# Two steps of an attention pair turned in one visit of TensorE, and five changes of order

## The chip, the cores and the metric

One core of a Trainium2 chip runs the whole program. The time is in microseconds (us) of the device for one execution. Lower is better. The engines are TensorE (PE, with its weight loads PEld), VectorE (DVE), ScalarE (ACT), GpSimd (POOL) and SyncE (SP), which only issues DMAs here.

## What is computed

```python
# attention: q, k, v are (4, 8, 576, 64); each position sees itself and the 63 before it
scores = np.matmul(q, k.transpose(0, 1, 3, 2)) / np.sqrt(D)
attn = softmax(np.where((rel >= 0) & (rel < 64), scores, -1e9))   # sum + 1e-9 below the line
x = np.matmul(attn, v)                                            # as 2304 tokens x 512
# first layer
x = ((x @ w1) * (x @ w2)) @ w3 @ w_out                            # 512 -> 1024 -> 1024 -> 512
# second layer
h = x @ w_in                                                      # 512 -> 2048
out = np.maximum(0.01 * h, h) @ w_out2                            # 2048 -> 512
```

## The kernel before

**Products.** w3 @ w_out is multiplied out first, so the first layer is two products, an elementwise one and a third. Every large product is cut into halves of both sides and done as seven block products P1 to P7 in place of eight, with sums of blocks before and behind. Each operand is split into a rounded part (hi, copied by ACT) and the rest (lo, subtracted by DVE), and a block product is three passes hi*hi, hi*lo, lo*hi (`three_passes`, lines 403 to 407). Tokens go in three chunks of 768.

**Stages.** The first stage makes w3 @ w_out in 16 slots (`wprod_slot`), each of 12 matmuls of 512 columns; its inputs come in pieces (`PIECES`), which ACT copies (`split_piece`, L818) and DVE subtracts (L1181). Then come 168 slots of the list `AB_SEQ`, twelve rounds r of 14 block products: slot n is one product of six matmuls of 384 columns (`ab_product`). `slot_of(r, m)` is the number of a slot; from round 1 on m runs from -1 to 12. Behind these come the third product of the first layer (`y_product`) and the two of the second layer.

**Attention** is laid between these slots. It has 36 steps g of 64 queries each, twelve per chunk; chunk 0 belongs to the first stage, chunk 1 to slots 5 to 47, chunk 2 to slots 62 to 104. Two steps, g even and g + 1, form a pair. In slots counted from the scores of a step (`SCORES[g]`, three slots between the steps of a pair, six from pair to pair), step g goes:
- scores of both steps of the pair on PE (L1695) at the end of the even one's slot;
- DVE scales and masks (L1225), and takes the row maximum (L1230), one slot later, for each step on its own;
- ACT's exponentials (L840) two and three slots later;
- DVE inverts the sums (`invert_sums`, L1240) four slots later, behind its work on that slot's product, and POOL multiplies the probabilities by them (`normalize`, L770);
- PE turns the probabilities with four transposes (`turn`, L1685) in the middle of the product eight slots later (`TURN`), into the bank `ps_more`; ACT copies them out (`turn_copy`, L834);
- PE multiplies with the values (`values`, L1675) for the pair, at the end of the slot nine behind the odd step's scores (`VALUES`), into the bank `ps_values`; ACT (in the first stage DVE) copies that out one slot later (`values_copy`).
In the first stage the numbers are 2 for the turn and 3 for the values.

**Order.** Each engine runs its instructions in the order in which the loops write them, and a wait on a semaphore holds everything behind it on that engine. There is no planner: the places of side work in slots are tables by hand (`AB_SUMS`, POOL's sums for weight unit f; `AB_HI` and `AB_LO`, ACT's and DVE's halves of the split of a unit; `XS_HI_NEXT` and `XS_LO_NEXT`, the same for blocks of x in rounds 4 and 8, where "t3" is a sum of x-parts on DVE). The banks of products are handed on by `bank_waits`: P6 waits for c11 (DVE, L1328), P2 for c21 of the round before (DVE, L1390). SP issues loads and stores in one queue; `store_p` and `store_p_late` write a round's three results.

Of the kernel before, what the change touches and what calls it, by code (L numbers as in the profile page):

```python
# [78 lines left out]
for _c in range(2):  # L79
    for _j in range(CSTEPS):  # L80
        SCORES[(_c + 1) * CSTEPS + _j] = slot_of(4 * _c, 5 + 3 * _j)
EXPS_A, EXPS_B, RECIP, TURN, VALUES = 2, 3, 4, 8, 9


SCORED, VALUED = {}, {}
for _g in range(NSTEP):
    SCORED[_g] = SCORES0[_g - _g % 2] if _g < CSTEPS else SCORES[_g - _g % 2]
    VALUED[_g] = SCORES0[_g | 1] + VALUES0 if _g < CSTEPS else SCORES[_g | 1] + VALUES

PIECES = []  # L90
# [33 lines left out]
def unit_of(f):  # L124
    if f < F_WSUM:
        return f
    if f < F_IN:
# [10 lines left out]
P0_HI = {2: (0, 0), 3: (0, 1), 5: (1, 0), 6: (1, 1), 9: (2, 0), 10: (2, 1), 12: (3, 0), 13: (3, 1)}  # L138
P0_LO = {3: (0, 0), 4: (0, 1), 6: (1, 0), 8: (1, 1), 10: (2, 0), 11: (2, 1), 13: (3, 0), 14: (3, 1)}
AB_LOAD = {(0, 2): (4,), (0, 6): (5,), (0, 10): (6,), (1, 1): (7,), (9, -1): (8, 9), (10, -1): (10, 11), (11, 8): (12, 13)}  # L140
AB_SUMS = {slot_of(0, 7): 4, slot_of(0, 10): 5, slot_of(1, 1): 6, slot_of(1, 4): 7}
AB_HI = {(1, 0): (4, 0), (1, 2): (4, 1), (1, 4): (5, 0), (1, 8): (5, 1),
# [3 lines left out]
AB_LO = {(1, 1): (4, 0), (1, 4): (4, 1), (1, 5): (5, 0), (1, 11): (5, 1),  # L146
# [3 lines left out]

XS_HI_FIRST = {2: P6, 3: P3, 4: P7, 7: P4}
XS_HI_LAST = {3: P2, 5: P1, 8: P5, 12: P6}
XS_HI_NEXT = {1: P3, 2: P7, 7: P4}
XS_LO_FIRST = {0: "t2", 1: "t3", 2: P6, 4: P3, 5: P7, 6: "t4", 8: P4}
XS_LO_LAST = {4: P2, 6: P1, 7: "t1", 9: P5, 11: "t2"}
XS_LO_NEXT = {-1: P6, 0: "t3", 3: P3, 4: P7, 5: "t4", 8: P4}

TYEARLY = 10
TY_LOAD = {(9, 6): (0, 1), (10, 3): (2, 3), (10, 8): (4, 5), (11, 2): (6, 7), (11, 5): (8, 9), (11, 9): (TYEARLY + 2,), (11, 11): (TYEARLY + 3,)}
# [56 lines left out]
def build(nc, qk_steps, v_steps, masks, w3, wo, w12, w_in, w_out, out):  # L216
    with ExitStack() as ctx:
# [75 lines left out]
        ps_scores = [ps_pair[:, :].rearrange("p (h b k) -> p h b k", h=HP, b=2)[:, :, b] for b in range(2)]  # L293
        ps_more = ctx.enter_context(nc.psum_tensor("ps_more", [P, 512], F32))
        ps_v = ctx.enter_context(nc.psum_tensor("ps_values", [P, 512], F32))
        ps_turned = ps_more[:, :].rearrange("p (h k) -> p h k", h=HP)
        ps_heads = ps_v[:, :].rearrange("p (h b q) -> p h b q", h=HP, b=2)

        wsum_dram = nc.dram_tensor("wsum_between", (KF, P, DM), F32, kind="Internal").ap()
# [23 lines left out]

        piece_in = [sem(f"piece_in{i}") for i in range(PRAW)]
        piece_hi = sem("piece_hi")
        piece_lo = sem("piece_lo")
        wprod_used = sem("wprod_used")
        wsum_done = [sem(f"wsum_done{i}") for i in range(4)]
# [80 lines left out]
        def bank(r, i, s):  # L409

            if r < AR:
                return (acc[s], acc[2 + s], acc[s], acc[s], acc[s], acc[2 + s], acc[s])[i]
            alpha = ((ps_s, ps_t), (acc[2], acc[3]))[r % 2][s]
            gamma, beta = (ps_v, ps_more)[s], acc[s]
            return (alpha, gamma, alpha, beta, alpha, gamma, alpha)[i]

        def piece_dest(i, part):

# [80 lines left out]
        def _(sp):  # L499
# [179 lines left out]
            for n in range(NSEQ):  # L679
                r = AB_SEQ[n][0]  # L680
                m = n - slot_of(r, 0)
                for g in range(CSTEPS + 2, NSTEP):
                    if SCORED[g - 2] == n - 1:
                        load_qk(g)
                    if VALUED[g - 2] == n - 1:
                        load_v(g)
                if r > 0 and m == 3:
                    store_p(r - 1)
                    store_p_late(r - 1)
                for f in AB_LOAD.get((r, m), ()):  # L690
                    load_fill(f)
                for u in range(NPRE):
                    if PRE_STORE[u] == n:
                        store_pre(u)
                    if PRE_LOAD[u] == n:
                        load_pre(u)
                for k in TY_LOAD.get((r, m), ()):
                    load_ty(k)
# [113 lines left out]
        def _(act):  # L812
# [18 lines left out]

            def turn_copy(g):
                act.wait_ge(turned, g + 1)
                act.activation(probs[g % 4], ps_turned, ACT.Copy).then_inc(pt_done, 1)  # L834

            def exps(g, pairs):
                r, w = g % 2, width(g)
# [134 lines left out]
            for i in (1, 3):  # L972
                act.dma_start(piece_raw[i], wo[PIECES[i][1]]).then_inc(piece_in[i], 16)
            act.dma_start(mask_s[:, :], masks).then_inc(mask_in, 16)
            for i in pieces_for(0):
                split_piece(i)
            for k in range(WSLOTS):
                for g in range(CSTEPS):
                    if SCORES0[g] + TURN0 == k - 1:
                        turn_copy(g)  # L980
                for i in pieces_for(k + 1):
                    split_piece(i)
                for g in range(CSTEPS):
                    if SCORES0[g] == k - 1:
                        exps(g, range(HP))
                if k in P0_HI:
                    split_fill(*P0_HI[k])
                if k == KF - 1:
                    save_wsum(0, 0)
                    save_wsum(0, 2)  # L990
                if k == WSLOTS - 5:
                    split_x(0, P2)
                if k == WSLOTS - 3:
                    split_x(0, P1)
# [4 lines left out]
            for n, (r, i, s) in enumerate(AB_SEQ):  # L999
                q, m = r // ROUNDS, n - slot_of(r, 0)  # L1000
                for g in range(CSTEPS, NSTEP):
                    if SCORES[g] + TURN == n:
                        turn_copy(g)
                    if g % 2 == 0 and VALUED[g] == n - 1:
                        values_copy(g)
# [170 lines left out]
        def _(dve):  # L1176
            dve.memset(probs[0][:, :, BQ:KW], 0.0).then_inc(probs_zero, 1)

            def split_piece(i):
                dve.wait_ge(piece_hi, i + 1)  # L1180
                dve.tensor_tensor(piece_dest(i, 1), piece_raw[i % PRAW], piece_dest(i, 0).bitcast(F32),  # L1181
                                  ALU.subtract).then_inc(piece_lo, 1)

# [275 lines left out]
                dve.tensor_tensor(lo, t_source(k), hi.bitcast(F32), ALU.subtract).then_inc(t_lo, 1)  # L1459


            for i in pieces_for(0):
                split_piece(i)
            for k in range(WSLOTS - 1):
# [201 lines left out]
        def _(pe):  # L1666
            def values(g):
                pe.wait_ge(v_in[g % 2], 16 * (g // 2 + 1))
                pe.wait_ge(pt_done, g + 1)
                pe.wait_ge(x_done, g - g % 2)  # L1670
                for h in range(H):
                    d = slice(h % 2 * D, (h % 2 + 1) * D)
                    w = slice(h * D, (h + 1) * D)
                    turned_at = (h ^ (h >= H // 2)) * BQ
                    last = pe.matmul(ps_heads[d, h // 2, g % 2], v_raw[:, g % 2, w],  # L1675
                                     pt[g % 4][:, turned_at:turned_at + BQ], start=True, stop=True)
                last.then_inc(values_done, 1)

            def turn(g):
                if g == 0:  # L1680
                    pe.wait_ge(probs_zero, 1)
                pe.wait_ge(probs_done, g + 1)
                pe.wait_ge(pt_done, g)
                for u in range(HP):
                    last = pe.transpose(ps_turned[:, u], probs[g % 4][:, u], ident[:, :])  # L1685
                last.then_inc(turned, 1)

            def scores(g):
# [10 lines left out]
            def attention_first(k):  # L1699
# [4 lines left out]
                    if SCORED[g] == k:  # L1704
                        scores(g)
                for g in range(CSTEPS):
                    if SCORES0[g] + TURN0 == k:
                        turn(g)

            def attention(n):  # L1710
# [6 lines left out]

            def first_slot():
                w, m_hi, m_lo = w3_ring[0], wo_s[:, 0, 0], wo_s[:, 0, 1]
                pe.wait_ge(piece_hi, 2)  # L1720
                for m in range(4):
                    pe.matmul(acc[m][:, :], w[:, 0, m * P:(m + 1) * P], m_hi, start=True, stop=False)
                    if m == 0:
# [58 lines left out]

            def turns(k):
                for g in range(CSTEPS, NSTEP):
                    if SCORES[g] + TURN == k:
                        turn(g)

            def ab_product(k, r, i, s):
# [161 lines left out]
```

## Time and profile before

| | us |
|---|---|
| median of 3 runs | 733.97 |
| lowest, highest | 733.32, 737.0 |
| the profiled execution, in all | 732.78 |
| its span in the trace | 730.9 |
| PE busy (share of the span) | 721.8 (99%) |
| PE's weight loads | 697.3 (95%) |
| DVE busy | 530.2 (73%) |
| ACT busy | 417.5 (57%) |
| POOL busy | 101.2 (14%) |
| granted clock of TensorE | 1.000 of full speed |

The span reaches from the first to the last instruction of the trace; the rest of the execution's time lies around it. PE's matmuls are shown with a modelled end, and one is shown as running when the next has begun: a row of 0.33 us is followed by the next start 0.17 us later. The starts, not the busy shares, tell whether PE lost time. Where a row ends with a bracket, the engine was idle for that long before it, and the name behind the arrow is what it waited for.

### The profile page before, as it was taken

To read this page: it belongs to the slowest core of one execution; us is meant where nothing else is said; L and a number is where in the kernel's file an instruction comes from. 1 tells how busy PE (TensorE), PEld (TensorE's weight loads), DVE (VectorE), ACT (ScalarE), POOL (GpSimd) and SP (SyncE) were. 2 spreads that over 40 slices of the span, in tenths; PEclk is the share of its full clock that TensorE was granted. 3 is DMA by queue.
4 is the path that set the end of the run, shared out by engine and by line. 5 is a ranking of instruction groups with operands and counts; after the bars stand their busy time and mean duration, and the time that the engine had idled before them with its cause. 6 is when DMAs were issued, how large, how long until landed. Compare 5 with 4: busy or idle time off the path is not lost.

```text
span 730.9 us, 13803 instructions
## 1 busy us (share of the span) xinstructions
PE 721.8 (99%) x5032; PEld 697.3 (95%) x5032; DVE 530.2 (73%) x833; ACT 417.5 (57%) x889; POOL 101.2 (14%) x122
## 2 busy tenths in 40 slices
PE   8999999999999999999999999999999999999998
PEld 7888899999899999999999999999999999999998
DVE  5988888797767679798778968669789655445452
ACT  5876677646564345656546656456677544544541
POOL 3433564413333110000000000000000000000000
DMA  9884677545654589988857988987996468778773
GB/s 324 296 300 164 208 233 239 190 163 183 197 172 172 184 300 393 313 279 322 296 178 291 323 281 295 359 285 248 377 375 244 130 181 241 206 215 232 207 202 116
DMA packets 96835, 181.13 MB, mean 248 GB/s; under 512 B 7936, under 2 KB 55680, under 8 KB 96768
## 3 DMA queue, kind: packets, MB, share of 16 engines
q1 hardware_dynamic: 90032, 166.62, 68.6%
q10 hardware_dynamic: 6736, 13.63, 5.2%
q8 instruction: 40, 0.66, 0.4%
q14 instruction: 27, 0.22, 0.1%
HBM read 111.80 MB, written 68.42 MB: 247 GB/s over the span
## 4 chain that ended last, share of the span: by engine, by line
PE 62%; ACT 0%; issue 0%; DVE 0%
PE acc L405 10%; PE acc L407 9%; PE acc L406 9%; PE ps_pair L405 5%; PE ps_pair L407 5%; PE ps_pair L406 5%; PE ps_more L407 3%; PE ps_more L405 3%; PE ps_values L405 3%; PE ps_values L407 3%; PE ps_more L406 3%; PE ps_values L406 3%; ACT arena L952 0%; DVE arena L1364 0%
## 5 line engine op out<-in xcount | busy, mean ns | idle before, releaser
L405 PE MATMUL acc<-parts,weights_a 128*128 128x384 f32 (+1 forms) x320 | 112.0, 350 | 0.9 <-DVE arena L1390 0.6
L407 PE MATMUL acc<-parts,weights_a 128*128 128x384 f32 (+1 forms) x320 | 109.5, 342 | 0.0
L405 PE MATMUL acc<-parts,weights_b 128*128 128x384 f32 x320 | 109.1, 341 | 0.3 <-DVE arena L1328 0.3
L406 PE MATMUL acc<-parts,weights_a 128*128 128x384 f32 (+1 forms) x320 | 109.3, 342 | 0.0
L407 PE MATMUL acc<-parts,weights_b 128*128 128x384 f32 x320 | 107.1, 335 | 0.0
L406 PE MATMUL acc<-parts,weights_b 128*128 128x384 f32 x320 | 107.0, 334 | 0.0
L1459 DVE TENSOR_TENSOR parts<-raw_c,parts 128x768 fp32r<-128x768 f32 x64 | 61.2, 958 | 60.2 <-ACT parts L957 60.1
L957 ACT ACTIVATE parts<-raw_c 128x768 fp32r<-128x768 f32 x64 | 54.0, 846 | 67.9 <-DMA raw_c<-g_between 65.5
L405 PEld LDWEIGHTS acc<-parts,weights_a 128*128 128x128 f32 x320 | 60.1, 188 | 5.2 <-issue 2.2
L840 ACT ACTIVATE arena<-arena,negmax 128x128 f32<-128x128 f32 (+1 forms) x144 | 55.2, 386 | 13.3 <-DVE negmax L1230 13.2
L405 PEld LDWEIGHTS acc<-parts,weights_b 128*128 128x128 f32 x320 | 60.1, 188 | 1.8 <-issue 1.2
L407 PEld LDWEIGHTS acc<-parts,weights_a 128*128 128x128 f32 x320 | 60.1, 188 | 1.7
L406 PEld LDWEIGHTS acc<-parts,weights_a 128*128 128x128 f32 x320 | 60.1, 188 | 1.3
L406 PEld LDWEIGHTS acc<-parts,weights_b 128*128 128x128 f32 x320 | 60.1, 188 | 0.0
L407 PEld LDWEIGHTS acc<-parts,weights_b 128*128 128x128 f32 x320 | 60.0, 188 | 0.0
L936 ACT ACTIVATE arena<-arena 128x384 f32<-128x384 f32 x72 | 35.9, 525 | 39.5 <-DVE arena L1328 17.6
L770 POOL TENSOR_TENSOR arena<-arena,rsum 128x512 f32<-128x512 f32 (+1 forms) x36 | 41.1, 1141 | 102.8 <-DVE rsum L1240 102.8
L911 ACT ACTIVATE parts<-arena 128x768 fp32r<-128x768 f32 x42 | 35.3, 848 | 33.9 <-PE ps_pair L407 11.5
L1400 DVE TENSOR_TENSOR parts<-arena,parts 128x768 fp32r<-128x768 f32 x42 | 39.7, 954 | 13.6 <-ACT parts L911 13.5
L1328 DVE TENSOR_TENSOR arena<-acc,arena 128x384 f32<-128x384 f32 x60 | 31.6, 552 | 17.2 <-PE acc L407 13.1
L405 PE MATMUL ps_pair<-parts,weights_b 128*128 128x384 f32 x120 | 40.1, 334 | 0.0
L406 PE MATMUL ps_pair<-parts,weights_b 128*128 128x384 f32 x120 | 40.1, 334 | 0.0
(212 smaller groups left out, 1761.9 us busy)
## 6 DMA issues: line engine op xcount, KB each, us to landing
g_between<-arena SPq DMA_DIRECT2D x75, 384.0 KB, 4.8
raw_c<-g_between SPq DMA_DIRECT2D x64, 384.0 KB, 3.4
arena<-p_between SPq DMA_DIRECT2D x42, 384.0 KB, 5.2
arena<-qk_steps SPq DMA_DIRECT2D x36, 384.0 KB, 5.0
arena<-v_steps SPq DMA_DIRECT2D x36, 256.0 KB, 3.8
p_between<-arena SPq DMA_DIRECT2D x24, 384.0 KB, 4.8
x_between<-arena ACTq DMA_DIRECT2D x21, 384.0 KB, 5.6
arena<-x_between SPq DMA_DIRECT2D x21, 384.0 KB, 5.6
```

Source lines behind the costliest of these rows:

```text
L405: eng.matmul(out_ap, w_hi, m_hi, start=start, stop=False, skip_group_check=resumed)
L406: eng.matmul(out_ap, w_hi, m_lo, start=False, stop=False, skip_group_check=resumed)
L407: return eng.matmul(out_ap, w_lo, m_hi, start=False, stop=stop, skip_group_check=resumed)
L770: pool.tensor_tensor(probs[g % 4][:, :, 0:w], probs[g % 4][:, :, 0:w], rsum[:, r * HP:(r + 1) * HP].unsqueeze(2).to_broadcast([P, HP, w]), ...
L840: act.activation(probs[g % 4][:, u, 0:w], probs[g % 4][:, u, 0:w], ACT.Exp, bias=negmax[:, r * HP + u:r * HP + u + 1], scale=1.0, accum_ou ...
L911: act.activation(block_places[k % NPROD][:, 0:BW], ty_raw[TY_SLOT[k]], ACT.Copy).then_inc(ty_hi, 1)
L936: act.activation(g, g, ACT.Prelu, alpha=SLOPE).then_inc(g_done[q], 1)
L957: act.activation(block_places[k % NPROD][:, 0:BW].rearrange("p (j t) -> p j t", j=2), t_source(k), ACT.Copy).then_inc(t_hi, 1)
L1328: dve.tensor_tensor(dest, bank(r, i, s)[:, 0:CT], p1_sb[:, s], ALU.add).then_inc(c11_done, 1)
L1400: dve.tensor_tensor(b[:, BW:2 * BW], ty_raw[TY_SLOT[k]], b[:, 0:BW].bitcast(F32), ALU.subtract).then_inc(ty_lo, 1)
L1459: dve.tensor_tensor(lo, t_source(k), hi.bitcast(F32), ALU.subtract).then_inc(t_lo, 1)
```

## The change

Both steps of a pair are turned in one visit of PE, in the slot that lies seven behind the odd step's scores (`TURNED`; in the first stage two behind, as before for the odd one). The even step goes to `ps_more` as before, the odd step to `ps_values`, so it waits until the values of the pair before have been copied out of there, and no longer until the even step's copy is done. The values of a pair wait for both copies. ACT copies the two one after the other. The slot of the values is the same.

Besides: POOL's sums for weight unit 5 move three slots back. In rounds 4 and 8 the sum "t3" on DVE moves from m = 0 to 2, and ACT's copy of block P7 from 2 to 3. DVE's parts (10, 1), (11, 0) and (11, 1) of the last weight splits move back. In round 5 SP issues `store_p` and `store_p_late` of the round before one slot later, behind loads. At the start DVE, in place of ACT, makes the hi part of the first piece of w_out.

```diff
-EXPS_A, EXPS_B, RECIP, TURN, VALUES = 2, 3, 4, 8, 9
+EXPS_A, EXPS_B, RECIP, TURN, VALUES = 2, 3, 4, 7, 9
+    TURNED[_g] = SCORES0[_g | 1] + TURN0 if _g < CSTEPS else SCORES[_g | 1] + TURN
@@ tables
-AB_SUMS = {slot_of(0, 7): 4, slot_of(0, 10): 5, slot_of(1, 1): 6, slot_of(1, 4): 7}
+AB_SUMS = {slot_of(0, 7): 4, slot_of(0, 13): 5, slot_of(1, 1): 6, slot_of(1, 4): 7}
-         (10, 6): (10, 0), (10, 11): (10, 1), (11, 1): (11, 0), (11, 4): (11, 1)}
+         (10, 6): (10, 0), (11, 1): (10, 1), (11, 4): (11, 0), (11, 5): (11, 1)}
-XS_HI_NEXT = {1: P3, 2: P7, 7: P4}
+XS_HI_NEXT = {1: P3, 3: P7, 7: P4}
-XS_LO_NEXT = {-1: P6, 0: "t3", 3: P3, 4: P7, 5: "t4", 8: P4}
+XS_LO_NEXT = {-1: P6, 2: "t3", 3: P3, 4: P7, 5: "t4", 8: P4}
@@ build
-        ps_turned = ps_more[:, :].rearrange("p (h k) -> p h k", h=HP)
+        ps_turned = [ps[:, :].rearrange("p (h k) -> p h k", h=HP) for ps in (ps_more, ps_v)]
+        def turned_place(g):
+
+            return ps_turned[g % 2]
@@ SP
-                if r > 0 and m == 3:
+                if r > 0 and m == (4 if slot_of(r, 3) in VALUED.values() else 3):
                     store_p(r - 1)
                     store_p_late(r - 1)
@@ ACT
-                act.activation(probs[g % 4], ps_turned, ACT.Copy).then_inc(pt_done, 1)
+                act.activation(probs[g % 4], turned_place(g), ACT.Copy).then_inc(pt_done, 1)
-            for i in pieces_for(0):
-                split_piece(i)
+            split_piece(0)
-                    if SCORES0[g] + TURN0 == k - 1:
+                    if TURNED[g] == k - 1:
-                    if SCORES[g] + TURN == n:
+                    if TURNED[g] == n:
                         turn_copy(g)
@@ DVE
-                dve.wait_ge(piece_hi, i + 1)
+                if i == 1:
+                    dve.wait_ge(first_hi, 1)
+                else:
+                    dve.wait_ge(piece_hi, max(i, 1))
+            dve.wait_ge(piece_in[1], 16)
+            dve.tensor_copy(piece_dest(1, 0), piece_raw[1]).then_inc(first_hi, 1)
             for i in pieces_for(0):
                 split_piece(i)
@@ PE, values
-                pe.wait_ge(pt_done, g + 1)
+                pe.wait_ge(pt_done, (g | 1) + 1)
@@ PE, turn
-                pe.wait_ge(pt_done, g)
+                if g % 2:
+                    pe.wait_ge(x_done, g - 1)
+                else:
+                    pe.wait_ge(pt_done, g)
@@ PE, first_slot
-                pe.wait_ge(piece_hi, 2)
+                pe.wait_ge(piece_hi, 1)
+                pe.wait_ge(first_hi, 1)
```

## Rows read from the trace of the kernel before

**Rows 1.** Windows: length, busy us of PE, PEld, DVE, ACT, POOL, clock, DMA share, GB/s.

```profile
140.00:190.00 50.00, 48.23 (x461) 45.41 (x460) 37.79 (x70) 26.91 (x81) 11.34 (x14) 1.00 0.58 191
```

**Rows 2.** Waits of PE: engine, tile and line, then releaser, total us, times, longest.

```profile
PE ps_more L1685 <- POOL arena L770: 1.1, 2, 0.9
```

**Rows 3.** Timeline of PE and ACT round one turn: start us, us, engine, line, operation.

```profile
120.18 0.34 PE L407 MATMUL acc<-parts,weights_b 128*128 128x384 f32 x1
120.36 0.60 PE L1685 MATMUL ps_more<-ident,arena 128*128 128x128 f32 x4
120.71 0.42 PE L405 MATMUL acc<-parts,weights_b 128*128 128x384 f32 x1
120.97 0.34 PE L406 MATMUL acc<-parts,weights_b 128*128 128x384 f32 x1
121.67 0.58 ACT L834 ACTIVATE arena<-ps_more 128x512 f32<-128x512 f32 x1
```

**Rows 4.** Timeline of DVE, POOL and PE round the turn of step 13.

```profile
88.18 0.18 DVE L1240 RECIPROCAL rsum<-sums_eps 128x4 f32<-128x4 f32 x1
89.97 1.35 POOL L770 TENSOR_TENSOR arena<-arena,rsum 128x512 f32<-128x512 f32 x1
90.12 0.34 PE L407 MATMUL acc<-parts,weights_a 128*128 128x384 f32 x1
91.37 0.66 PE L1685 MATMUL ps_more<-ident,arena 128*128 128x128 f32 x4 [0.92 <-POOL arena L770]
```

**Rows 5.** Timeline of DVE, POOL and PE round the turn of step 15.

```profile
99.10 1.20 DVE L1193 TENSOR_TENSOR weights_b<-raw_b,weights_b 128x1024 fp32r<-128x1024 f32 x1
99.27 1.93 POOL L770 TENSOR_TENSOR arena<-arena,rsum 128x512 f32<-128x512 f32 x1 [0.34 <-DVE rsum L1240]
99.72 0.33 PE L407 MATMUL acc<-parts,weights_a 128*128 128x384 f32 x1
100.76 0.34 PE L407 MATMUL acc<-parts,weights_a 128*128 128x384 f32 x1
```

**Rows 6.** Timeline of POOL and PE round the turn of step 33.

```profile
209.42 1.04 POOL L770 TENSOR_TENSOR arena<-arena,rsum 128x512 f32<-128x512 f32 x1 [6.27 <-DVE rsum L1240]
211.09 0.60 PE L1685 MATMUL ps_more<-ident,arena 128*128 128x128 f32 x4
```

**Rows 7.** Timeline of PE at two turns of the first stage.

```profile
28.60 0.60 PE L1685 MATMUL ps_more<-ident,arena 128*128 128x128 f32 x4
29.17 0.50 PE L405 MATMUL acc<-parts,weights_a 128*128 128x512 f32 x1
```

**Rows 8.** Timeline of DVE and PE, sixth product of round 4.

```profile
154.99 0.95 DVE L1274 TENSOR_TENSOR arena<-arena 128x768 f32<-128x768 f32 x1
155.96 0.34 PE L407 MATMUL acc<-parts,weights_a 128*128 128x384 f32 x1
156.55 0.41 PE L405 MATMUL acc<-parts,weights_a 128*128 128x384 f32 x1 [0.25 <-DVE arena L1328]
```

**Rows 9.** Timeline of SP's DMA issues and of PE, scores of steps 30 and 31.

```profile
174.68 0.57 SPq L588 DMA_DIRECT2D p_between<-arena  x1
179.40 1.00 SPq L573 DMA_DIRECT2D arena<-qk_steps  x2
186.22 0.67 PE L1695 MATMUL ps_pair<-arena 64*64 64x128 f32 x16 [1.52 <-DMA arena<-qk_steps]
```

**Rows 10.** Timeline of DVE and PE, third product of round 11.

```profile
275.43 1.21 DVE L1193 TENSOR_TENSOR weights_b<-raw_b,weights_b 128x1024 fp32r<-128x1024 f32 x1
276.19 0.34 PE L407 MATMUL acc<-parts,weights_a 128*128 128x384 f32 x1
277.17 0.44 PE L405 MATMUL acc<-parts,weights_a 128*128 128x384 f32 x1 [0.64 <-DVE arena L1390]
```

**Rows 11.** Timeline of DVE and PE at the first products.

```profile
5.48 0.69 DVE L1181 TENSOR_TENSOR weights_a<-arena,weights_a 128x512 fp32r<-128x512 f32 x1 [4.35 <-ACT weights_a L818]
6.36 0.39 PE L1725 MATMUL acc<-parts,weights_a 128*128 128x512 f32 x1
```

More of the change, by code:

```diff
@@ L81 @@
         SCORES[(_c + 1) * CSTEPS + _j] = slot_of(4 * _c, 5 + 3 * _j)
-EXPS_A, EXPS_B, RECIP, TURN, VALUES = 2, 3, 4, 8, 9
-SCORED, VALUED = {}, {}
+EXPS_A, EXPS_B, RECIP, TURN, VALUES = 2, 3, 4, 7, 9
+SCORED, TURNED, VALUED = {}, {}, {}
 for _g in range(NSTEP):
     SCORED[_g] = SCORES0[_g - _g % 2] if _g < CSTEPS else SCORES[_g - _g % 2]
+    TURNED[_g] = SCORES0[_g | 1] + TURN0 if _g < CSTEPS else SCORES[_g | 1] + TURN
     VALUED[_g] = SCORES0[_g | 1] + VALUES0 if _g < CSTEPS else SCORES[_g | 1] + VALUES
@@ L325, in build @@
         piece_hi = sem("piece_hi")
+        first_hi = sem("first_hi")
         piece_lo = sem("piece_lo")
@@ L1682, in turn @@
                 pe.wait_ge(probs_done, g + 1)
-                pe.wait_ge(pt_done, g)
+                if g % 2:
+                    pe.wait_ge(x_done, g - 1)
+                else:
+                    pe.wait_ge(pt_done, g)
                 for u in range(HP):
-                    last = pe.transpose(ps_turned[:, u], probs[g % 4][:, u], ident[:, :])
+                    last = pe.transpose(turned_place(g)[:, u], probs[g % 4][:, u], ident[:, :])
                 last.then_inc(turned, 1)
@@ L1706, in attention_first @@
                 for g in range(CSTEPS):
-                    if SCORES0[g] + TURN0 == k:
+                    if TURNED[g] == k:
                         turn(g)
@@ L1784, in turns @@
                 for g in range(CSTEPS, NSTEP):
-                    if SCORES[g] + TURN == k:
+                    if TURNED[g] == k:
                         turn(g)
```

## The prediction

> **What bounds the kernel now.** I read the stages first, then who made PE wait, then starts on PE's timeline. The windows show PE busy for 48.23 of 50 us in one of the slices with attention work, clock 1.00, nothing else near full [rows 1]: TensorE's own stream is the bound. A matmul's shown length overlaps the next one, so I don't count busy time but starts: two third passes of neighbouring products begin at 99.72 and 100.76, so **a product costs 1.04 us**, 0.173 us a matmul [rows 5]. Every start later than that pace is a stall of the whole kernel. Going through all starts up to 290 us I find eight stalls in the stages that overlap products with attention, 5.1 us together, and some 0.9 us in the first stage; behind 290 us ten short ones sum to 1.0, and the change touches none of them. The wait list names POOL's normalisation twice [rows 2].
>
> **The turn visits.** A visit of four transposes costs: the pass before starts at 120.18, the second after it at 120.97, which is 0.79 us, less two passes (0.35), so 0.44 [rows 3]. Four transposes at 0.11 are that already; entering and leaving cost about 0.02. Twenty-four visits in the product stages become twelve, so joining them gives 12 x 0.02 = **-0.2 us** (between 0 and 18 x 0.1 = 1.8, were the entry as dear as the 0.1 that a visit of values or scores loses on entering; the transposes' own row is the nearer, so 0.2). The same eight transposes are still made.
>
> **The odd step comes one product earlier.** TURN was 8 slots behind each step's own scores; now both go 7 behind the odd one's. The even one gains two slots, the odd one loses one, 1.04 us. The 0.44 of the even transposes was ahead of the odd ones before as well, only elsewhere, so the odd turn is wanted at its old time less 1.04. It needs the normalised probabilities. What sets those is not PE: DVE combines the product of slot +4, masks the next even step, inverts the sums, and then POOL multiplies. Nothing of that moves. So I compare for each odd step the end of POOL's instruction plus 0.05 for the semaphore with the old start less 1.04:
> Step 13: turn wanted at 90.12 + 0.17 = 90.29, it came at 91.37 because POOL ended at 91.32 [rows 4]. POOL was late because sums of a weight unit stood ahead of it; these move three slots back. The reciprocal was ready at 88.18 + 0.18 = 88.36 [rows 4], so POOL ends at about 88.4 + 1.3 = 89.7; wanted at 89.25: a stall of 0.5 in place of 1.08.
> Step 15: wanted at 100.76 + 0.17 - 1.04 = 99.89, POOL ends at 99.27 + 1.93 = 101.20 [rows 5]: 1.36 (was 0.32).
> Step 33: wanted at 211.09 - 1.04 = 210.05, POOL ends at 210.46 [rows 6]: 0.46.
> The same subtraction for the twelve odd steps 13, 15, ... 35 gives 0.5, 1.36, 0.19, 1.09, 0.47, 0.21, 0.75, 0, 0.72, 0.47, 0.46, 0; ten of twelve stall, **+6.2 us**. The instruction behind is on PE itself: the second half of a product, and all products after it; there is no later point at which PE gets the time back, since PE is the bound. The bounds: with every full-width multiplication at its shortest, 1.04 [rows 6], the sum is 3.6; with every one at the 1.93 of step 15 [rows 5] it is 13.0. I take the measured length of each, as DVE's and POOL's orders there are unchanged.
> That length is a matter of company. At step 15 DVE's subtraction with both inputs in SBUF runs from 99.10 to 100.30, POOL's multiplication from 99.27 takes 1.93 [rows 5] against 1.04 [rows 6]. The Trainium skill, SBUF — State Buffer, section Who interferes with whom, says that of a DVE instruction with two SBUF inputs and a GpSimd instruction that reads SBUF the one that starts second is blocked until the other is done. By that rule, the trace agrees here, and a POOL that started ahead of DVE at every odd step would give the 3.6 of the lower bound.
>
> **What else waits on the new visit.** ACT copies both turned steps back to back, 0.58 us each [rows 3]. The copy of the slot's product stands behind them, but that product is itself later by the same transposes, so it starts about 0.1 us late as before; the tightest user, the next product into that bank, comes a whole product later, 0.3 us in hand: nothing. The values need both copies at 2.5 slots, 2.6 us: nothing. If ACT were a full copy behind, 0.3 at one of twelve visits. The new wait of the odd turn for its bank (ps_values, read out one slot behind the values): that copy ends 1.9 to 3.4 us before the turn in the first stage, and three slots before it later: nothing. What it would queue is again PE's whole stream.
>
> **First stage.** There the odd turn stays and the even one is joined to it, so no probability is wanted earlier. ACT's mid-slot wait for the even turn goes, and behind that wait stood the copies of the next weight pieces. At 28.60 a visit takes 0.57 to the next matmul at 29.17 where 0.35 is the usual [rows 7]: 0.22 of waiting for a piece whose first copy stood behind turn_copy. Of four such stalls (0.16, 0.22, 0.35, 0.16) I count 0.16 + 0.22 + 0.15: the third is mostly a PSUM copy behind four exponentials, the fourth DVE's own backlog. **-0.5** (0 to 0.9).
>
> **The five mends.** (a) POOL's sums later: the 1.08 and 0.32 of steps 13 and 15 are in the subtraction above as removed, -1.40. (b) A sum of x-parts (0.95 us) held DVE from 154.99 while P6 waited for c11: 156.55 against 155.96 + 0.17, 0.42 [rows 8]; the same in round 8, 0.43. Moved two slots, its next user is the fourth block at slot +8, with 0.4 us in hand: -0.85. (c) SP issued three stores from 174.68 and the loads of q and k of steps 30 and 31 only at 179.40; PE's second half of the scores came at 186.22 [rows 9], 1.66 late. With the loads first they go as soon as the scores before them are done, three us earlier, and even at the 6.2 us that the late one took they land by 182.4: -1.66. The stores are 1.3 us later, and their next user is over two slots off. (d) DVE's subtraction of 1.21 us at 275.43 stood ahead of p21, and P2 began at 277.17 instead of 276.36: 0.81 [rows 10]. It moves to where c11 follows within 0.15 us: -0.8 (0.6 if c11 is next late). A wait of 0.26 for c11 in round 2 is swallowed by the new stall of step 19 one slot earlier. Together 1.40 + 0.85 + 1.66 + 0.81 + 0.26 = **-4.98**.
> (e) The first piece of wo is copied by DVE beside ACT. PE's first matmul no longer waits for ACT's second copy, but its second matmul, at 6.36, needs DVE's subtraction of 0.69, which ran from 5.48 [rows 11] and is now behind DVE's copy of a piece that landed at about 5.0. A copy of this size lasts between 0.3 and 0.69, so the subtraction starts at 5.3 to 5.7, and the second matmul at 6.2 to 6.4: **-0.07**.
>
> **Sum:** 6.2 - 4.98 - 0.5 - 0.2 - 0.07 = **+0.45 us**. The profiled execution took 732.78 us in all, 730.9 of it span; the median of the three runs is 733.97, 1.2 above. I add the sum to the median: **734.4**.
>
> **Rivals.** A, the forecast: mends pay, the odd turns take it back; 734.4, chance 0.58.
> B, hollow mends: behind (c) and (d) stands another wait of the same size, for instance the transfers, as DMA is busy 0.58 on average there and far more round the stall [rows 1]. Against it: the loads are small and slack is 1.6 us. +1.66 + 0.81: 736.9, chance 0.14.
> C, the normalisation is quick: POOL gets ahead of DVE at the odd steps and the stalls sum to 3.6. For it: three of the full-width odd steps already show 1.04. Against it: what DVE does beside POOL is the same work in the same order. 731.8, chance 0.14.
> D, no odd stalls at all, because the chain ahead of POOL also comes earlier by a slot: 734.4 - 6.2 = 728.2. Against it: DVE's step there begins with a product that PE has just finished. Chance 0.07.
> E, slower: at all full-width steps POOL is blocked as at step 15, stalls of 13.0 in place of 6.2: 734.4 + 6.8 = 741.2. It decides for slower once the stalls sum to more than 9.4, 0.8 a visit. Against it: only steps 15 and 19 took over 1.4. Chance 0.07.
>
> **How the numbers follow.** About 0.5% (3.7 us) is what a measurement of this kernel tells from no change. A, B and C lie within it: 0.86; D is faster, 0.07; E slower, 0.07. The range takes in B and C with 1 us of scatter: 730.8 to 738.1; D and E lie outside.
>
> **What would show it.** In the changed profile: waits of PE's transposes on POOL's multiplication rise from 2 to about ten, 5 to 6 us in all; the waits on q and k, on p21 and on c11 of rounds 4 and 8 are gone; visits of eight transposes last 0.87 us where nothing waits. I am wrong if the odd transposes follow the even ones without a gap, or if PE's idle in 140:190 does not fall although (c) is gone.

## The result and the profile after

The changed kernel takes 738.05 us (736.48 to 739.42), the kernel before 734.85 us on the same chip (731.98 to 737.0), 20 runs of each: ratio **1.0051, interval 1.004 to 1.0061**. The forecast was 734.4 and "no change"; the kernel is slower by 3.2 (medians) to 3.7 us (ratio), just inside the end of the range (738.1).

The profiled execution of the changed kernel took 738.78 us (span 736.7), 6.0 more than that of before (732.78). Medians differ by about half of that: before's profiled run was a short one, and after's a little longer than its median. What follows explains the pair of profiles first and says what of it the medians keep.

The waits of PE in the changed kernel (line and tile, releaser, total us, times, longest):

```profile
PE ps_values L1698 <- POOL arena L776: 5.7, 8, 2.2
PE ps_pair L407 <- ACT arena L904: 0.6, 1, 0.6
PE acc L407 <- DVE arena L1398: 0.5, 1, 0.5
PE acc L407 <- DVE arena L1346: 0.5, 1, 0.5
PE ps_pair L1708 <- DMA arena<-qk_steps: 0.2, 1, 0.2
```

L1698 is the turn, L776 POOL's multiplication. Two waits on it, 1.1 us, have become eight, 5.7 us [rows 2]; the forecast said about ten, 5 to 6 us. (One more wait, 1.5 us at the start, is in before as well and is left out here.) The wait on q and k has shrunk to 0.2. Three more, on DVE L1398, ACT L904 and DVE L1346, are in the slots 142, 184 and 264, which the change doesn't edit.

Step 13 and step 33 (start, us, engine, line, operation), which answer to [rows 4, 6]:

```profile
87.67 1.04 POOL L776 TENSOR_TENSOR arena<-arena,rsum 128x512 f32<-128x512 f32 x1 [2.18 <-DVE rsum L1248]
88.08 0.60 PE L1698 MATMUL ps_more<-ident,arena 128*128 128x128 f32 x4
88.76 0.66 PE L1698 MATMUL ps_values<-ident,arena 128*128 128x128 f32 x4
...
213.99 1.04 POOL L776 TENSOR_TENSOR arena<-arena,rsum 128x512 f32<-128x512 f32 x1 [6.57 <-DVE rsum L1248]
214.15 0.60 PE L1698 MATMUL ps_more<-ident,arena 128*128 128x128 f32 x4
215.09 0.66 PE L1698 MATMUL ps_values<-ident,arena 128*128 128x128 f32 x4 [0.33 <-POOL arena L776]
```

The odd transposes could begin 0.44 behind the even ones. At step 33 they begin at 215.09 and not at 214.59: POOL ends at 215.03, and PE stands for **0.50 us** (0.46 was forecast). At step 13 it stands for 0.24 (0.5 forecast).

Step 15, which answers to [rows 5]:

```profile
98.14 0.60 PE L1698 MATMUL ps_more<-ident,arena 128*128 128x128 f32 x4
98.30 0.18 DVE L1248 RECIPROCAL rsum<-sums_eps 128x4 f32<-128x4 f32 x1
98.40 3.27 DVE L1201 TENSOR_TENSOR weights_b<-raw_b,weights_b 128x1024 fp32r<-128x1024 f32 x2
98.83 2.02 POOL L776 TENSOR_TENSOR arena<-arena,rsum 128x512 f32<-128x512 f32 x1
100.90 1.12 PE L1698 MATMUL ps_values<-ident,arena 128*128 128x128 f32 x4 [2.16 <-POOL arena L776]
102.14 0.52 PE L408 MATMUL acc<-parts,weights_a 128*128 128x384 f32 x1
102.46 0.52 PE L409 MATMUL acc<-parts,weights_a 128*128 128x384 f32 x1
```

PE is ready for the odd step at 98.58 and begins at 100.90: **2.32 us** where 1.36 was forecast. DVE starts its two subtractions at 98.40, POOL its multiplication at 98.83, and that takes 2.02 in place of 1.04. Then something appears that the trace of before has nowhere: the matmuls behind the stall follow each other at 0.32, not at 0.17. The windows (length, busy us of PE, PEld, DVE, ACT, POOL, clock, DMA share, GB/s) name it:

```profile
98.00:100.00 2.00, 0.74 (x6) 0.47 (x4) 1.97 (x5) 1.77 (x6) 1.92 (x3) 1.00 0.99 379
100.00:102.00 2.00, 1.10 (x5) 1.10 (x6) 2.00 (x2) 1.47 (x6) 2.00 (x2) 0.68 1.06 396
102.00:104.00 2.00, 2.00 (x8) 2.00 (x7) 1.24 (x4) 1.58 (x5) 1.84 (x4) 0.50 0.56 178
104.00:106.00 2.00, 2.00 (x23) 1.75 (x24) 0.87 (x2) 1.99 (x7) 1.57 (x2) 0.97 0.00 0
...
140.00:190.00 50.00, 48.74 (x465) 45.94 (x463) 39.59 (x71) 27.71 (x82) 14.47 (x18) 1.00 0.58 186
```

**TensorE runs at half clock** (1.2 in place of 2.4 GHz) from the end of the stall on. The clock lost is (1 - 0.68) x 2 + (1 - 0.50) x 2 + (1 - 0.97) x 2 = 1.7 us, so it was 3.4 us at half clock. The last row is the one that answers to [rows 1]: PE busy rises from 48.23 to 48.74, since two odd stalls (0.58 and 1.00) stand there in place of the waits for c11 and for q and k (0.42 and 1.66).

The mends that pay, in the same order as before's rows [rows 8 to 10]:

```profile
160.24 0.33 PE L409 MATMUL acc<-parts,weights_a 128*128 128x384 f32 x1
160.42 0.33 PE L407 MATMUL acc<-parts,weights_a 128*128 128x384 f32 x1
...
180.72 0.37 SPq L579 DMA_DIRECT2D arena<-qk_steps  x1
189.05 1.10 PE L1708 MATMUL ps_pair<-arena 64*64 64x128 f32 x32
...
281.64 0.33 PE L409 MATMUL acc<-parts,weights_a 128*128 128x384 f32 x1
281.82 0.33 PE L407 MATMUL acc<-parts,weights_a 128*128 128x384 f32 x1
```

P6 of round 4 starts at the pace (0.18 behind the pass before it), the scores of 30 and 31 run through in one piece of 32, and P2 of round 11 doesn't wait for p21.

**Where the time went**, as the start of a product after the change less its start before, from PE's timelines:

```
slot            5     17     20     24     47     62     81    104    119    143    157    end
after - before -0.73 -1.57 -1.84 +2.18 +4.28 +3.86 +3.26 +5.08 +4.57 +5.39 +4.53 +5.83
```

The whole loss of the first stretch is made between slots 20 and 24: 4.0 us, of which 2.0 are the stall (2.32 for 0.32) and 1.7 the half clock; the rest is four transposes that before had ahead of slot 20. From 24 to 47 and 81 to 104 the other odd steps add 2.1 and 1.8. The falls are the mends: -0.42 at slot 62, -1.76 at 81, -0.43 at 118, -0.81 at 156. The rises at slots 142 (0.70), 184 (0.73) and 264 (0.59) are the late waits named above, 2.0 us together. Before's profiled run had none of them. Those at 184 and 264 are of different size from profile to profile, and the kernel with the joined turns alone (e2, next section), which has none of the five changes of order, has both (1.02 and 0.80). So they hang on neither half alone, and I take them for a matter of the execution: they are 1.3 us that the pair of profiles exaggerates.

The one at 142 is another matter. P2 waits there for c21, and c21 stands behind a subtraction for the weights. First before, then after:

```profile
259.61 1.21 DVE L1193 TENSOR_TENSOR weights_b<-raw_b,weights_b 128x1024 fp32r<-128x1024 f32 x1
260.97 0.56 DVE L1390 TENSOR_TENSOR arena<-acc,arena 128x384 f32<-128x384 f32 x1
...
265.33 1.22 DVE L1201 TENSOR_TENSOR weights_b<-raw_b,weights_b 128x1024 fp32r<-128x1024 f32 x1
266.46 0.55 DVE L1398 TENSOR_TENSOR arena<-acc,arena 128x384 f32<-128x384 f32 x1
267.06 0.44 PE L407 MATMUL acc<-parts,weights_a 128*128 128x384 f32 x1 [0.54 <-DVE arena L1398]
```

PE is 4.57 us later here, the subtraction 5.72. All eleven profiled kernels that have the changes of order lose time at this place, 0.2 to 0.9 us (1.4 in one), and the two that don't have them, before and e2, lose none. So this wait goes with the changes of order, though none of their edits lies next to it; why ACT's copy ahead of that subtraction comes later there was not tested.

### The profile page after: what moved, and what is told of

Its sections match the earlier page's. It is cut to its first block, busy times and chain, and to the rows that moved or that the text cites. A ratio compares the mean times of both kernels' runs of the same rounds, so it can differ in the third digit from the quotient of the medians.

```text
span 736.7 us, 13804 instructions
## 1 busy us (share of the span) xinstructions
PE 724.5 (98%) x5032; PEld 699.3 (95%) x5032; DVE 531.4 (72%) x834; ACT 415.6 (56%) x888; POOL 101.2 (14%) x122
## 4 chain that ended last, share of the span: by engine, by line
PE 56%; DMA 2%; ACT 1%; DVE 1%; issue 0%; ACTq 0%; DVEq 0%; SPq 0%
PE acc L407 8%; PE acc L408 8%; PE acc L409 8%; PE ps_pair L407 5%; PE ps_pair L408 5%; PE ps_pair L409 5%; PE ps_more L408 3%; PE ps_values L408 3%; PE ps_more L409 3%; PE ps_values L407 3%; PE ps_more L407 3%; PE ps_values L409 3%; DMA x_between<-arena 1%; DMA p_between<-arena 1%; DMA arena<-p_between 1%
## 5 line engine op out<-in xcount | busy, mean ns | idle before, releaser
L776 POOL TENSOR_TENSOR arena<-arena,rsum 128x512 f32<-128x512 f32 (+1 forms) x36 | 40.9, 1137 | 106.6 <-DVE rsum L1248 106.6
```

The source lines that it names most:

```text
L776: pool.tensor_tensor(probs[g % 4][:, :, 0:w], probs[g % 4][:, :, 0:w], rsum[:, r * HP:(r + 1) * HP].unsqueeze(2).to_broadcast([P, HP, w]), ...
```

## The experiments

Each ratio is to the kernel before, run beside it on the same chip.

**Which half of the change costs.** The five changes of order alone, and the joined turns alone.

```diff
@@ e1_mends_only: the kernel before and
+AB_SUMS, AB_LO, XS_HI_NEXT, XS_LO_NEXT, SP's order and first_hi as in the change
@@ e2_pair_only: the kernel before and
-EXPS_A, EXPS_B, RECIP, TURN, VALUES = 2, 3, 4, 8, 9
+EXPS_A, EXPS_B, RECIP, TURN, VALUES = 2, 3, 4, 7, 9
+    TURNED[_g] = SCORES0[_g | 1] + TURN0 if _g < CSTEPS else SCORES[_g | 1] + TURN
+            return ps_turned[g % 2]
```

> The kernel before with the five changes of order alone; turns as before. Theory 1 (the changes of order pay, and the odd turn one product earlier takes it back): 1.4 us of POOL waits, 0.85 of c11 waits, 1.66 of the q and k load, 0.8 of p21 and 0.1 at the start go, 4.8 us less than the kernel before, ratio 0.9935. Theory 2 (joining the turns costs in itself, wherever it stands): the same 0.9935. Theory 3 (other waits take the place of those removed): within 1.5 us of the kernel before, ratio 0.998 to 1.000.

> The joined turns alone, seven slots behind the odd scores, without the five changes of order. Theory 1: the stalls of the odd turns, with POOL's sums still ahead of step 13, are 7.8 us in place of 1.4 + 0.26, less 0.5 in the first stage, plus about 1 us of half clock on the mean: 6.5 us more than before, ratio 1.009. Theory 3: the changes of order were worth nothing, so the same as the changed kernel, ratio 1.005.

Measured: 731.58 us, ratio 0.9962 (0.9946 to 0.9977), and 740.38 us, 1.0075 (1.0049 to 1.0101). The mends are worth 2.5 (medians) to 2.8 us (ratio), not 4.98; the joined turns cost 5.5 to 6.3, near the +5.5 of the forecast's 6.2 - 0.5 - 0.2. That nearness is partly luck, as the measured time has in it the half clock, which the forecast lacked. In the joined kernel the half clock appears behind step 13, which there stalls for 2.1 us. In the other, the stall of step 13 is gone and that of step 15 has grown:

```profile
98.97 2.02 POOL L771 TENSOR_TENSOR arena<-arena,rsum 128x512 f32<-128x512 f32 x1
101.04 0.66 PE L1690 MATMUL ps_more<-ident,arena 128*128 128x128 f32 x4 [1.54 <-POOL arena L771]
```

In start times: 1.14 us gained at step 13, and 1.38 given back at step 15, in one place. So the shape of the answer was there at once: what TensorE gains ahead of step 15, it waits for at step 15.

**Is mend (a) worth anything?** The same kernel with POOL's sums of unit 5 back at slot 10.

```diff
-AB_SUMS = {slot_of(0, 7): 4, slot_of(0, 13): 5, slot_of(1, 1): 6, slot_of(1, 4): 7}
+AB_SUMS = {slot_of(0, 7): 4, slot_of(0, 10): 5, slot_of(1, 1): 6, slot_of(1, 4): 7}
```

> The five changes of order without the one on POOL (its sums for unit 5 stay ahead of step 13). If gains ahead of step 15 are worth nothing, since its probabilities come at 101 us in every kernel: the same as with it, ratio to before 0.996, a stall of 1 us at step 13 and one of under 0.5 at step 15. If the forecast's 1.4 us were right: 1.4 us slower, ratio 0.998.

Measured: 731.29 us, 0.9949 (0.9929 to 0.9968), not to be told from 731.58. The stalls are 1.1 at step 13 and 0.3 at step 15 as in [rows 4, 5], and the trace is 0.65 us *ahead* of the kernel with the mend at slot 23 (0.25 of that from the start). Among single turns the 1.40 of mend (a) was worth nothing.

**Is it the early odd turn?** The changed kernel with the joined visit one slot later, for all pairs and for the pair 14/15 alone.

```diff
@@ e3_pair_at8
-EXPS_A, EXPS_B, RECIP, TURN, VALUES = 2, 3, 4, 7, 9
+EXPS_A, EXPS_B, RECIP, TURN, VALUES = 2, 3, 4, 8, 9
@@ e4_pair3_at8
-    TURNED[_g] = ... else SCORES[_g | 1] + TURN
+    TURNED[_g] = ... else SCORES[_g | 1] + TURN + (_g in (14, 15))
```

> The changed kernel with the joined visit one slot later: TURN 8, the odd step where it was in the kernel before. Theory 1: no probability is wanted earlier, PE's waits on POOL are at most 0.5 us, clock 1.000 in every run, the changes of order and the first stage keep their 5.3 us: ratio 0.993. Theory 2: the double copy and the second bank cost, and now with a slot less before the values: at least as slow as the changed kernel, ratio 1.005 or more. Theory 3: ratio 1.000.

> The changed kernel with the joined visit of steps 14 and 15 alone one slot later. Theory 1 (the long stall of step 15, 2.3 us, is what brings the half clock behind it): the stall falls to 1.3 or less and the clock is 1.000 in every run: 1.0 us of stall and on the mean 0.9 of half clock less than the changed kernel, ratio to before 1.0025. Rival (the half clock has another cause, or comes with any of the later stalls of 0.5 to 1 us): clock 0.997 to 0.998 in about half of the runs as in the changed kernel, ratio 1.004.

Measured: 732.94 us, 0.9981 (0.9968 to 0.9994), and 735.92, 1.0022 (1.0007 to 1.0037). One slot later for all takes 5.1 us off the changed kernel, and the trace loses its stalls step by step as the forecast's subtraction has them. One pair alone takes 2.1 off: its stall goes from 2.3 to 1.3, and the clock behind it is full. But e3 is still 1.4 us behind the mends alone, and its trace has two waits that those lack: P6 of round 2 for c11 (0.5) and a product of round 5 for ACT's copy of the product before it (0.6):

```profile
PE acc L407 <- ACT arena L886: 0.4, 1, 0.4
PE acc L407 <- DVE arena L1336: 0.4, 1, 0.4
```

Joining by itself has a price, where I had said "nothing".

**Is it DVE that holds POOL at step 15?** The changed kernel with two of DVE's subtractions two products later.

```diff
-AB_LO = {(1, 1): (4, 0), (1, 4): (4, 1), (1, 5): (5, 0), (1, 11): (5, 1),
+AB_LO = {(1, 1): (4, 0), (1, 6): (4, 1), (1, 7): (5, 0), (1, 11): (5, 1),
```

> The changed kernel with one change: two of VectorE's subtractions for the weights (of units 4 and 5) in round 1 are done two products later, so that none of them runs beside GpSimd's multiplication of step 15. Theory, that this multiplication ends late because VectorE's two-input subtraction holds it (2.02 us for 1.04) and that VectorE has no pause from 87 to 102 us: the multiplication takes 1.0 to 1.4 us, TensorE's stall at step 15 falls from 2.3 to 1.3 to 1.7 us, the 3.4 us at half clock behind it are gone, and the time is 735.3 to 736.3 us, ratio 1.001 to 1.003 against 1.005. Rival, that GpSimd's own queue (the sums of unit 6 ahead of it) is what counts: the multiplication ends at 100.8 as before, stall 2.3 us, half clock, 1.005. A third: the subtractions, moved, hold VectorE's product sums and the multiplication of step 16 or 17, and a stall of 0.5 us or more appears there.

Measured: 735.94 us, 1.0018 (1.0006 to 1.0029), 2.1 us less than the changed kernel (2.4 by the ratios).

```profile
98.51 0.60 PE L1698 MATMUL ps_more<-ident,arena 128*128 128x128 f32 x4
98.77 0.68 DVE L1233 SCALAR_TENSOR_TENSOR arena<-ps_pair,arena 128x512 f32<-128x512 f32 x1
99.19 1.04 POOL L776 TENSOR_TENSOR arena<-arena,rsum 128x512 f32<-128x512 f32 x1
100.28 0.66 PE L1698 MATMUL ps_values<-ident,arena 128*128 128x128 f32 x4 [1.17 <-POOL arena L776]
...
96.00:106.00 10.00, 8.83 (x104) 7.78 (x104) 8.03 (x15) 8.45 (x26) 9.50 (x10) 1.00 0.80 264
```

With the mask beside it the multiplication takes 1.04, the stall is 1.33, and the clock stays at 1.00. POOL's own queue still sets its start (99.19, behind its sums of unit 6), but not its length; the stall of the first rival (2.3 us) didn't come. No new stall at step 17; step 19's stayed at 0.89.

**Is the half clock a thing of the stall's length?** The mends alone, with PE's turn of step 15 held until POOL's next sum is done, by which the stall goes from 1.7 to 3.2 us by the starts and nothing else is moved.

```diff
+                if g == 15:
+                    pe.wait_ge(w12_s1, 8)
```

> The five changes of order alone, and the turn of step 15 made to wait for one more instruction of POOL, so that PE's stall there grows from 1.5 to 3.1 us and nothing else is changed. Theory 1 (one stall of over 2 us is what the clock answers to): besides the 1.6 us the clock is at half for some 3.4 us in most runs, clock 0.998, 3.3 us more than the five changes alone: ratio to before 1.0005. Rival (the half clock in the changed kernel comes of something else): clock 1.000, 1.6 us more: ratio 0.998.

Measured: 734.36 us, 0.9996 (0.9981 to 1.0011), 2.8 us over the mends alone (2.5 by the ratios) for 1.5 us of added waiting.

```profile
102.93 0.63 PE L1692 MATMUL ps_more<-ident,arena 128*128 128x128 f32 x4 [2.99 <-issue]
103.91 0.52 PE L408 MATMUL acc<-parts,weights_a 128*128 128x384 f32 x1
104.22 0.52 PE L406 MATMUL acc<-parts,weights_a 128*128 128x384 f32 x1
...
104.00:106.00 2.00, 2.00 (x8) 1.84 (x6) 0.56 (x1) 2.00 (x10) 1.92 (x3) 0.50 0.01 4
```

Here no turn is joined, and the pitch is again 0.31 to 0.32 at a granted clock of 0.50. Nine of twelve runs have a clock under 1 (median 734.9), the three others took 732.4, 733.2 and 733.5. Of the mends alone one of twelve is under 1, at 0.999. So a stall of this kind brings the half clock in most executions, and 1.7 us with it. In the changed kernel ten of 20 runs are at 0.997 or 0.998, which is what 3.4 us at half clock make of the mean (median 738.6 against 737.15 of the rest). A run at 0.999 need not have had it: in the profiles of e3 and e4 (0.9996 and 0.9995) the half clock lies in the last 3 us, when TensorE has nothing left to do.

The kernel before isn't free of it either: of its 69 runs beside the experiments 14 are at 0.997 or 0.998 (medians 735.97 against 734.05). Of the 82 runs of the nine kernels that have the mends and no stall of over 1.8 us, none is. So what the changed kernel adds over before is less than its own share; the clocks of before's 20 runs beside it are not on record.

**Does it help to serve POOL first?** DVE inverts the sums ahead of masking the next step, in the changed kernel and in the mends alone.

```diff
                 for g in range(CSTEPS, NSTEP):
+                    if SCORES[g] + RECIP == n:
+                        invert_sums(g)
+                for g in range(CSTEPS, NSTEP):
                     if SCORES[g] == n - 1:
                         mask_scores(g)
-                for g in range(CSTEPS, NSTEP):
-                    if SCORES[g] + RECIP == n:
-                        invert_sums(g)
```

> The changed kernel with DVE's inversion of the sums put ahead of the masking of the next step in the same slot, so that every odd step's probabilities come 1.4 us earlier. Theory 1 (the odd turns wait for the chain mask, inversion, POOL): PE's waits on POOL fall from 5.7 us to under 1, the clock is 1.000, 6 us of stall and 0.9 of half clock less than the changed kernel: ratio to before 0.9945. Theory 2 (the joined visit costs in itself, by ACT's two copies in a row): the waits on POOL go, but others take their place: ratio 0.999 or more.

> The five changes of order alone, with the inversion ahead of the masking. Theory 1: the one stall left, 1.5 us at step 15, where DVE works without a pause, goes: 1.5 us less than the five changes alone, ratio to before 0.994. Rival (the stall at step 15 is POOL's multiplication being blocked by DVE's subtraction, and the order of DVE does not matter): ratio 0.996, stall over 1 us.

Measured: 732.11 us, 0.9963 (0.9948 to 0.9978), and **730.30 us, 0.9941 (0.9921 to 0.9961)**, the shortest kernel of the study and faster than both. Step 15 in the first of them:

```profile
97.59 1.04 POOL L776 TENSOR_TENSOR arena<-arena,rsum 128x512 f32<-128x512 f32 x1 [0.32 <-DVE rsum L1248]
98.61 0.60 PE L1698 MATMUL ps_more<-ident,arena 128*128 128x128 f32 x4
99.05 0.60 PE L1698 MATMUL ps_values<-ident,arena 128*128 128x128 f32 x4
```

POOL starts 1.2 us earlier and ahead of the subtraction, and the odd transposes follow 0.44 behind the even ones; no wait on POOL is left. That order takes some 6 us off the changed kernel (738.05 to 732.11), and 1.3 off the mends alone. With all such waits gone the joined kernel is still 1.8 us longer than the one with single turns.

**Where does that rest come from?** First, ACT's two copies put behind its copy of the slot's product; then the joined visit in the first stage alone.

```diff
@@ e9_after_inv_late_copy
-                for g in range(CSTEPS, NSTEP):
-                    if TURNED[g] == n:
-                        turn_copy(g)
                 ...
                 if i == P4 and s == 0:
                     copy_a21(r)
+                for g in range(CSTEPS, NSTEP):
+                    if TURNED[g] == n:
+                        turn_copy(g)
@@ e10_inv_first_stage_pair
+    TURNED[_g] = SCORES0[_g | 1] + TURN0 if _g < CSTEPS else SCORES[_g] + TURN + 1
```

> The changed kernel with the sums inverted ahead of the mask (as e5), and in the rounds ScalarE's two copies of the turned steps put behind its copy of the slot's product instead of ahead of it. Double copy ahead of the product copy (theory): with the row after it waited 0.7 us on ScalarE's copy (PE acc L407 <- ACT arena L886) and a little in slot 17, TensorE gets back 0.5 to 1.1 us: ratio to before 0.9948 to 0.9956 against e5's 0.9963, 730.7 to 731.3 us, and the 0.7 us row is gone. Rival, that joining costs because TensorE must stand for the odd step whatever ScalarE does: the time of e5 stays, 0.996 to 0.997, and the copies, now later, make the values wait (PE ps_values on ACT, 0.4 us or more).

> The changes of order and the sums inverted ahead of the mask (as e6), and the two steps of a pair turned in one visit only in the first stage; in the rounds the odd step is turned a product later, as before. If the joined visits of the first stage are worth what the prediction said (0.5 us) and the loss of e5 against e6 comes from the rounds alone: 729.8 us, ratio 0.9935 (0.992 to 0.995), the shortest yet. Rival, that the first stage's gain is eaten at step 13 or 15, where VectorE's chain sets the end and not TensorE: the same as e6, 0.9941 within 0.0005, and the first stage's gain seen in the trace up to slot 14 is gone by slot 22.

Measured: 730.96 us, 0.996 (0.9945 to 0.9975), and 730.73 us, 0.995 (0.9934 to 0.9966). Against 0.9963 and 0.9941 neither can be told from no change. Both medians come from another chip than e5's and e6's, so only the ratios compare. The traces say more than the times. Among PE's waits in e5 stand these two:

```profile
PE acc L407 <- ACT arena L886: 0.7, 1, 0.7
PE ps_values L1685 <- issue: 0.4, 1, 0.4
```

With the copies behind, the first is gone (-0.82 at slot 74), and the second, the values of step 14 behind their copy, has grown from 0.6 to 1.0 us by the starts (+0.54 at slot 24). Both theories hold, each at its own place, and the sum stays open. With only the first stage joined (e10 against e6), PE is 0.31 us behind at w1, the second of the first stage's 16 slots, before any joined visit, and 0.07 ahead at the stage's end: 0.38 gained for the 0.5 forecast. The 0.07 is still there behind step 15 (0.06 at slot 24), so the gain isn't given back at that step when POOL has been served first. It doesn't show in the total, because later waits differ by as much: at slot 140 e10 is 0.26 behind, at 142 it is 0.40 ahead, where e6 waits 0.85 and e10 0.20. Counted in the same way, from w1 to w15 against the 57.4 us of single turns, the eight profiles with a joined first stage gain 0.03 to 0.37, the changed kernel 0.20.

## Why the prediction was wrong

**The odd turns: right in kind and nearly in sum.** Ten of twelve were to stall, 6.2 us together. The distances in the trace are 0.24, 2.32, 0.21, 0.89, 0.50, 0.58, 1.00, 0, 0.74, 0.50, 0.50, 0: ten stall, 7.5 us. Without step 15 it is 5.2 against 4.9. Moving all visits back by a slot took off 5.1 us of the median.

**Step 15: the term that failed, and mend (a) with it.** The forecast held POOL's end at 101.20, and that was nearly right: 100.85. But the time at which PE wants the step, 99.89, was read on before's time axis, where the 1.08 of step 13 still stands, which the same sum had just taken out, and the 0.5 of the first stage too. PE was ready at 98.58, 1.31 us earlier, and POOL's end came 0.35 earlier: 1.36 + 1.31 - 0.35 = 2.32, the stall that was measured. DVE works without a gap from about 87 to 102 us, and POOL takes its turn behind DVE's inversion and its own sums, not behind PE; so what PE gains ahead of this point it waits for here. Among single turns that is shown: without mend (a) the time is the same (e8), its 1.40 were worth nothing. In the changed kernel it wasn't taken out; there the joined turns without it have their long stall at step 13 instead (e2).

**The half clock: a term that was missing.** 1.7 us in the executions that have it, and these are ten of 20, so some 0.9 us on average; against before, which has it in some executions too (14 of the 69 beside the experiments, some 0.3 us on average) it is nearer 0.5. The windows of before showed 1.00 everywhere that I read, its longest stall there being 1.7 us, and I took a stall to cost only its own length. The Trainium skill, TensorE: Matmul & The Clock Gate, Part 1, says that the array's clock is halved once TensorE has been idle for a while; the traces agree, in that 2.3 us (after) and 3.2 us (e7) of standing have 3.4 us at half clock behind them, and 1.3 (e11) and 1.7 (e1) have none.

**ACT's double copy: "nothing" was wrong.** With all waits on POOL gone, the joined kernel is 1.8 us behind the single one (732.11 and 730.30), and 1.4 in the pair e3 and e1. I had compared the product's copy with its tightest user and found 0.3 in hand; at slot 74 that user waited 0.7, and the values of step 14 waited 0.6 for the second copy, which I had given 2.6 us. Both are shown by rows; that they are the whole of the 1.8 is not, since moving the copies only traded the one for the other.

**The single mends.** (b) 0.42 + 0.43, (c) 1.76 and (d) 0.81 came as costed (0.85, 1.66, 0.81), and none had another wait close behind it. Rival B, hollow mends, was right for the one mend that it did not name, (a), and in part by the wait at slot 142, which takes 0.2 to 0.9 us back (1.4 once) in every kernel with the mends. Of (e) and the first stage, 0.73 us are seen at slot 5 against 0.57 forecast, but 0.5 of that is the start, and it includes an input that landed at 4.08 in place of 4.97 us. The rows show how it goes now: DVE's copy takes 0.43, its first subtraction ends at 5.29.

```profile
4.11 0.43 DVE L1471 CAST parts<-arena 128x512 fp32r<-128x512 f32 x1 [2.98 <-DMA arena<-wo_tiles]
4.60 0.69 DVE L1189 TENSOR_TENSOR weights_a<-arena,weights_a 128x512 fp32r<-128x512 f32 x1
```

The joined visit itself is as told: at 28 us the second four follow 0.43 behind the first, and the next matmul 0.36 behind those, where it was 0.57 [rows 7].

```profile
27.91 0.60 PE L1698 MATMUL ps_more<-ident,arena 128*128 128x128 f32 x4
28.34 0.60 PE L1698 MATMUL ps_values<-ident,arena 128*128 128x128 f32 x4
28.70 0.48 PE L407 MATMUL acc<-parts,weights_a 128*128 128x512 f32 x1
```

**Slower, but not by the rival that I wrote for it.** Rival E wanted POOL to be blocked at every odd step; it was blocked long at two (2.02 at step 15, 1.71 at step 19). The sum as it should have stood: +0.45, +1.3 for the stalls (1.0 of it step 15), +0.5 for the half clock over before's own, +0.3 for the first stage and +0.7 for slot 142, as it was in the profiled run: 3.2 or 3.3, against 3.2 to 3.7 in the medians. It is put together afterwards, from terms of single traces, so its closeness proves little. In the pair of profiles it is 0.45 + 1.3 + 1.7 + 0.3 and the 2.0 of late waits, 5.75 for 5.83. What ACT's double copy costs in the changed kernel itself can't be read off: its stalls on POOL hide those waits, and they show only where the stalls are gone. The single mends sum to 3.4 in the traces and the mends alone to 2.5 to 2.8 in the medians; the wait at slot 142 takes back 0.59 in that trace, but the half clock of before, which the mends' runs don't have, should add some 0.3, so a part of the difference stays open. Open too is why the wait at 142 comes, and how much of the waits at 184 and 264 an average execution of before has.

## What to carry to other kernels

Before booking the removal of a stall as a gain, ask which engine sets the next wait of the bottleneck engine, and whether that engine moves too: a chain on another engine that has no pause is a fixed date, and everything gained ahead of it is waited for there. When a queue of one engine feeds another that feeds the bottleneck, do the small step that the far one waits for first: here 0.3 us of sums ahead of 1.4 us of masking removed every wait on POOL that the change had brought. And price a stall by more than its length where the bottleneck is TensorE: a long one may be followed by a stretch at half clock.

## What the hardware showed

- A stall of 2.1 to 3.2 us was followed by 3.4 us at half clock in the profiles of after, e2 and e7 (granted 0.50, matmuls of 384 columns 0.32 apart in place of 0.17), 1.7 us of work; not in every run (10 of 20, 4 of 6, 9 of 12), and in no profile behind stalls of 1.3 to 1.7 us. What decides in one run and not in another was not tried.
- POOL's multiplication of 128x512 with a DVE subtraction of two SBUF inputs begun before it took 2.02 us, with the mask or nothing beside it 1.04; moving the subtraction away made the one into the other (e11).
- The kernel before has runs with a clock of 0.997 or 0.998 too, 8 of 22 in one set; none of these was profiled, so where their stall lies stays open. The kernels with the changes of order and no long stall have none in 82 runs; whether the 1.66 us wait for q and k, which those changes remove, is what brings it in before was not tested.
